# Unread constant products on TensorE at the start and in the slots of two stages, shorter rotary tables, a rotated bank ring

## The reference

```python
# q, k, v: (4, 8, 576, 64); each head of each batch:
q_rot, k_rot = rotate(q), rotate(k)                  # rotary embedding with cos and sin
scores = scale * q_rot @ k_rot.T
attn = exp(scores - max(scores)); attn = attn / (sum(attn) + 1e-9)
attn_out = attn @ v
# x: (4, 576, 512), the heads side by side
h = x.transpose(0, 2, 1) @ U @ V                     # U: (576, 32), V: (32, 576)
u = x + h.transpose(0, 2, 1)
out = u + relu(u @ w_ch1) @ w_ch2                    # 512 -> 2048 -> 512
```

## Time and profile before

| | us |
|---|---|
| median of 3 runs | 759.92 (759.8 to 761.0) |
| profiled execution, device time | 758.6 |
| its span, first to last instruction | 756.8 |
| PE busy | 714.9 |
| POOL, ACT, DVE busy | 464.9, 439.3, 405.3 |

### The profile page before, as it was taken

The page is one execution under the profiler, slowest core; times in us unless marked ns, Lnnn a source line. Parts: engine busy times, 40 slices in busy tenths (PEclk is TensorE's granted clock), DMA queues, the critical chain, the costliest instruction groups (busy, mean ns, idle before and its releaser), DMA issues.

```text
span 756.8 us, 12306 instructions
## 1 busy us (share of the span) xinstructions
PE 714.9 (94%) x4292; PEld 644.6 (85%) x4292; DVE 405.3 (54%) x675; ACT 439.3 (58%) x948; POOL 464.9 (61%) x338
## 2 busy tenths in 40 slices
PE   3999977899999989999999999989999999999998
PEld 3888875798998879899999988879899889999986
DVE  4799977655556775443454466666565441112111
ACT  2788865666666665565565665657656443334341
POOL 3998846485849663674855957638432446565653
PEclk9999999999999999999999999999999999999999
DMA  7976682627383528448275274372612254434341
GB/s 206 239 215 183 174 250 74 199 87 227 102 254 105 167 94 240 155 130 258 81 213 183 96 197 146 117 211 69 169 70 98 70 195 137 166 127 169 128 169 72
DMA packets 73964, 118.11 MB, mean 156 GB/s; under 512 B 27056, under 2 KB 27184, under 8 KB 72112
## 3 DMA queue, kind: packets, MB, share of 16 engines
q1 hardware_dynamic: 73472, 116.68, 50.9%
q10 hardware_dynamic: 432, 0.66, 0.3%
HBM read 80.45 MB, written 9.44 MB: 119 GB/s over the span
## 4 chain that ended last, share of the span: by engine, by line
PE 75%; DVE 9%; ACT 7%; issue 5%; DMA 1%; POOL 1%; SPq 0%; POOLq 0%; ACTq 0%; DVEq 0%
PE ps L1129 25%; PE ps L1145 23%; PE ps L1043 8%; PE ps L1029 8%; PE ps L1063 6%; DVE negmax L863 3%; ACT prob L711 2%; PE ps L1056 1%; DVE ptl L872 1%; PE ps L1021 1%; DMA raw<-in_qk 1%; DVE pth L876 1%; ACT low L728 1%; PE ps L1086 1%; ACT pth L722 1%
## 5 line engine op out<-in xcount | busy, mean ns | idle before, releaser
L647 POOL TENSOR_TENSOR w2l<-w2u,w2h 128x512 fp32r<-128x512 f32 x96 | 123.8, 1290 | 227.4 <-ACT w2h L775 227.4
L964 DVE SCALAR_TENSOR_TENSOR htl<-ps,hth 128x384 fp32r<-128x384 f32 x96 | 53.5, 558 | 184.8 <-ACT hth L782 184.5
L863 DVE TENSOR_REDUCE negmax<-ps 128x1 f32<-128x576 f32 (+1 forms) x160 | 120.2, 751 | 56.4 <-PE ps L1029 46.6
L722 ACT ACTIVATE pth<-ps 128x512 fp32r<-128x512 f32 x156 | 87.8, 567 | 87.1 <-PE ps L1063 85.3
L711 ACT ACTIVATE prob<-ps,negmax 128x576 f32<-128x576 f32 (+1 forms) x160 | 118.1, 738 | 33.9 <-DVE negmax L863 32.4
L1129 PE MATMUL ps<-ub,w1h 128*128 128x384 f32 x384 | 132.3, 344 | 1.8 <-DVE utl L955 1.8
L1129 PE MATMUL ps<-ub,w1l 128*128 128x384 f32 x384 | 129.4, 337 | 0.0
L1129 PE MATMUL ps<-utl,w1h 128*128 128x384 f32 x384 | 129.2, 336 | 0.0
L641 POOL TENSOR_TENSOR w1l<-w1u,w1h 128x512 fp32r<-128x512 f32 x96 | 123.6, 1288 | 6.7 <-ACT w1h L771 6.7
L782 ACT ACTIVATE hth<-ps 128x384 fp32r<-128x384 f32 x96 | 47.1, 491 | 137.6 <-PE ps L1129 137.3
L1029 PE MATMUL ps<-stack 128*128 128x288 f32 x620 | 114.4, 307 | 9.3 <-ACT prob L711 9.0
(11 more groups left out here) (80 smaller groups left out, 1128.1 us busy)
## 6 DMA issues: line engine op xcount, KB each, us to landing
w1u<-in_w SPq DMA_DIRECT2D x96, 256.0 KB, 2.6
w2u<-in_w SPq DMA_DIRECT2D x96, 256.0 KB, 2.7
stack<-raw SPq DMA_DIRECT2D x60, 288.0 KB, 4.5
raw<-in_qk SPq DMA_DIRECT2D x14, 1152.0 KB, 5.4
stack<-raw SPq DMA_DIRECT2D x60, 144.0 KB, 3.9
v2u<-in_v SPq DMA_DIRECT2D x16, 320.0 KB, 3.8
ubu<-scratch_u SPq DMA_DIRECT2D x18, 256.0 KB, 3.7
out<-ubu SPq DMA_DIRECT2D x18, 256.0 KB, 2.2
```

Source lines behind the costliest of these rows:

```text
L647: nc.gpsimd.tensor_tensor(w2l[:, at], w2u[:, at], w2h[:, at], ALU.subtract).then_inc(w2_lo, 1)
L722: nc.scalar.activation(pt_of(g)[0][rows, keys, queries], source, ACT.Copy).then_inc(pt_hi, 1)
L863: nc.vector.tensor_reduce(negmax[0:WT[t], t:t + 1], scores_of(n, WT[t]), AX.XY, ALU.max, negate=True).then_inc(maxed, 1)
```

## The change

It has five parts. (1) Ahead of everything TensorE waits for a DVE memset of `hsum` and makes six 128x512 products of it into bank 7, which nobody reads; the wait for the identity comes after them. (2) In slots 1 to 7 and 47 to 55 two products of the identity with itself (128x128, plain fp32) are made into the first score bank, after the wait for that bank and ahead of the scores, which overwrite them. (3) The tables come as one DMA of 64 partitions, and DVE copies them to the other 64. SP issues q and k of round 1 and v of round 0 at once, with no wait, ahead of head 1's operands; k of round 1 has a semaphore of its own. POOL begins the product of round 1's q as soon as the tables are doubled and q is loaded, and waits for DVE's two splits after that product. (4) `RING_MIXED` is rotated by one bank. (5) LAGGED is 51.

```diff
+WARM_UP = 6
+FILLED, FILLERS = (*range(1, 8), *range(47, 56)), 2
-MERGED, LAGGED, MLP_FROM = 46, 50, 56
+MERGED, LAGGED, MLP_FROM = 46, 51, 56
-RING_ALONE, RING_MIXED, RING_MERGED = (4, 5, 6, 7), (4, 5, 6, 7, 2, 3), (6, 7)
+RING_ALONE, RING_MIXED, RING_MERGED = (4, 5, 6, 7), (5, 6, 7, 2, 3, 4), (6, 7)
             sp.dma_start(raw[:, 0, :, 0], qk[0][:, :, 0]).then_inc(raw_loaded[0], 16)
-            sp.wait_ge(raw_loaded[0], 16)
             sp.dma_start(raw[:, 1, :, 0], qk[1][:, :, 0]).then_inc(raw_loaded[1], 16)
+            sp.dma_start(raw[:, 1, :, 1], qk[1][:, :, 1]).then_inc(next_k, 16)
+            load_v(0)
             sp.wait_ge(lo_split[1], 1)
             stack_k(sp, 0, 1)
             sp.wait_ge(lo_split[0], 1)
             stack_q(sp, 0, 1)
-            sp.dma_start(raw[:, 1, :, 1], qk[1][:, :, 1]).then_inc(first_loaded, 16)
-            load_v(0)
             load_v(1)
                 link(nc.gpsimd.tensor_tensor(both, both, tables[:, :, :], ALU.mult))
+                if r == 1 and which == 0:
+                    for i in range(2):
+                        pool.wait_ge(lo_split[i], 1)
                 nc.gpsimd.tensor_tensor(both[:, 0], both[:, 0], both[:, 1], ALU.add).then_inc(roped[which], 1)
-            pool.wait_ge(tables_loaded, 32)
-            for which in range(2):
-                pool.wait_ge(lo_split[which], 1)
+            pool.wait_ge(tables_twice, 1)
-            act.dma_start(tables[:, 0], cos).then_inc(tables_loaded, 16)
-            act.dma_start(tables[:, 1], sin).then_inc(tables_loaded, 16)
+            act.dma_start(tables[0:D], trig).then_inc(tables_loaded, 16)
-            dve.wait_ge(tables_loaded, 32)
+            nc.vector.memset(hsum[:, :], 1.0).then_inc(filled, 1)
+            dve.wait_ge(tables_loaded, 16)
+            nc.vector.tensor_copy(tables[D:P], tables[0:D]).then_inc(tables_twice, 1)
+            dve.wait_ge(tables_twice, 1)
+            pe.wait_ge(filled, 1)
+            for _ in range(WARM_UP):
+                nc.tensor.matmul(ps[:, 7 * BANK:8 * BANK], hsum[:, 0:P], hsum[:, :], start=True, stop=True)
             pe.wait_ge(ident_loaded, 16)
+            def fill(at):
+                for _ in range(FILLERS):
+                    nc.tensor.matmul(ps[:, at:at + P], ident[:, :], ident[:, :], start=True, stop=True)
                 at = 2 * BANK * (n % 2 if n < MERGED else 0)
+                if n in FILLED:
+                    fill(at)
```

More of the change, by code:

```diff
@@ L284, in _down_read, with build @@
         eng.wait_ge(e["down_done"], i + 1 - p)
-def build(nc, qk, v, cos, sin, identity, u4, v4, w, scratch_u, out):
+def build(nc, qk, v, trig, identity, u4, v4, w, scratch_u, out):
     out = out.rearrange("b s d -> (b s) d")
@@ L335, in build @@
         vmraw = lu[:, :, :].rearrange("p x n -> p (x n)")[:, 0:S]
-        tables_loaded, ident_loaded = sem("tables_loaded"), sem("ident_loaded")
+        tables_loaded, ident_loaded, filled = sem("tables_loaded"), sem("ident_loaded"), sem("filled")
+        next_k, tables_twice = sem("next_k"), sem("tables_twice")
         first_loaded, mix_loaded, mix_consts = sem("first_loaded"), sem("mix_loaded"), sem("mix_consts")
@@ L366, in _engines @@
 def _engines(nc, e):
-    (qk, v, cos, sin, identity, u4, v4, w, scratch_u, out, bank_of, before, left) = (e[x] for x in (
-        "qk v cos sin identity u4 v4 w scratch_u out bank_of before left").split())
+    (qk, v, trig, identity, u4, v4, w, scratch_u, out, bank_of, before, left) = (e[x] for x in (
+        "qk v trig identity u4 v4 w scratch_u out bank_of before left").split())
     (ps, ident, tables, raw, first, stack, v2u, v2, prob, pth, ptl, low, xt, negmax, sums, inv, xn, xh, xl, hsum, hs, us, vs,
@@ L372, in _engines @@
          "uth utl w1h w1u w1l w2h w2u w2l hth htl res uraw vmraw pt_buffers").split())
-    (tables_loaded, ident_loaded, first_loaded, mix_loaded, mix_consts, zeroed, raw_loaded, v_loaded, first_rope,
+    (tables_loaded, ident_loaded, filled, next_k, tables_twice, first_loaded, mix_loaded, mix_consts, zeroed, raw_loaded, v_loaded, first_rope,
      chain, roped, qk_hi, lo_split, v_hi, v_split, stacked, scored, maxed, expd, transposed, pt_hi, pt_lo, pv_done,
@@ L377, in _engines @@
      relu_lo, down_done, acc_done, added, res_loaded, stored) = (e[x] for x in (
-         "tables_loaded ident_loaded first_loaded mix_loaded mix_consts zeroed raw_loaded v_loaded first_rope "
+         "tables_loaded ident_loaded filled next_k tables_twice first_loaded mix_loaded mix_consts zeroed raw_loaded v_loaded first_rope "
          "chain roped qk_hi lo_split v_hi v_split stacked scored maxed expd transposed pt_hi pt_lo pv_done "
@@ L605, in prepare @@
                     if r == 1:
-                        pool.wait_ge(first_loaded, 32)
+                        pool.wait_ge(next_k, 16)
                     rope(r, 1)
@@ L1212 @@
     s = np.sin(freqs).T.astype(np.float32)
-    c = np.concatenate([c] * 4, axis=0)
-    s = np.concatenate([-s, s] * 2, axis=0)
+    c = np.concatenate([c] * 2, axis=0)
+    s = np.concatenate([-s, s], axis=0)
     root = np.float32(D ** -0.25)
-    cos = np.ascontiguousarray(c * root)
-    sin = np.ascontiguousarray(s * root)
-    arrays = {"qk": qk, "v": vp, "cos": cos, "sin": sin, "identity": np.eye(P, dtype=np.float32),
+    trig = np.ascontiguousarray(np.stack([c * root, s * root], axis=1))
+    arrays = {"qk": qk, "v": vp, "trig": trig, "identity": np.eye(P, dtype=np.float32),
               "u4": u4, "v4": v4, "w": w}
@@ L1223 @@
     out = nc.dram_tensor("out", (B, S, DM), my.dt.float32, kind="ExternalOutput").ap()
-    build(nc, aps["qk"], aps["v"], aps["cos"], aps["sin"], aps["identity"], aps["u4"], aps["v4"], aps["w"],
+    build(nc, aps["qk"], aps["v"], aps["trig"], aps["identity"], aps["u4"], aps["v4"], aps["w"],
           scratch_u, out)
```

## The result

The changed kernel takes 763.09 us (median of 9 runs, 762.2 to 764.9), the kernel before 760.04 us beside it (median of 9, 759.4 to 762.1). The ratio is 1.005, with a 95% interval of 1.0036 to 1.0063: 3 us slower, where 753.5 us was forecast. The profiled execution took 762.95 us, its span is 761.1 us. That of the kernel before (758.6 us) was 1.4 us under its median, so the profiles lie 4.3 us apart where the medians lie 3.05 us apart.

A forecast was written before the change was run, and what follows sets the result against it. TensorE bounds from 142 us, DVE from about 37 us to slot 46, TensorE's low clock before. 758.6 - 2.7 (start) - 3.1 (middle) = 752.8 us; as a median 754.1, taken as 753.5, range 749.5 to 757.5.

The forecast's parts named there:

- The clock in slots 1 to 7: Head 0's slots: TensorE runs at 2.4 instead of 1.2 GHz, so a slot takes 1.68 instead of 2.78 us.
- The slower rival, C: Slots 1 to 7 stay at 1.2 GHz, seven pairs cost 6.2 us: 761 us, 763 with POOL in the way; chance 0.07.
- the loads: At the start: one table DMA less brings products 1 and 0 forward by 0.8 us.
- the middle: Slots 46 to 55: 2.9 + 0.5 - 0.3 = 3.1 us gained, between 1 and 4.
- POOL against DVE: Start: POOL's early product delays a DVE step, first maximum at 14.2 instead of 11.7 us, 2.5 us given back.
- The price of the unread products: On TensorE: a pair costs 0.44 us at 2.4 GHz, twice that at 1.2; the six at the start some 9 us.
- The gain at the high clock: Start to slot 12: 5.2 us gained in all, 1.4 of it by the first maximum, before POOL's delay.
- POOL isn't late: Heads 2 and 3: after DVE's splits POOL does what it did before, less the 2.62 us product of q.
- Slot 46, the ring: TensorE's 3.20 us idle wait for bank 4 goes; the maximum of slot 47 moves from 103.17 to 100.3, 2.9 us.
- Slots 47 to 55: DVE is nearer to being the bound, TensorE's room takes most pairs; 0.3 us charged for all nine.
- LAGGED: Slot 51: the 0.69 us `hsum` step moves from ahead of the maximum to behind it, 0.5 us gained.
- start: Up to slot 12: 2.7 us gained with POOL's product in DVE's way, 5.2 without.

The follow-up runs named there:

- e1: The changed kernel with POOL's waits for DVE's two splits put back ahead of POOL's first product; 760.69 us, ratio 1.0001 to the kernel before.
- e5: e1 with nine instead of six unread products at the start; 754.54 us, ratio 0.9935.
- e10: e7 without the pairs of unread products in slots 1 to 7, so nine products at the start and no pairs; 754.8 us, ratio 0.9919.
- e11: e6 with the pairs of unread products in slots 47 to 55 alone; 757.85 us, ratio 0.9969.
- e4: The changed kernel without the six products at the start and the pairs in slots 1 to 7; late pairs stay; 758.77 us, ratio 0.9985.
- e7: e5 without the pairs of unread products in slots 47 to 55; 754.26 us, ratio 0.9930.
- e6: The changed kernel without any unread products and with POOL's waits as in e1; 754.0 us, ratio 0.9935.
- e2: The kernel before with RING_MIXED rotated by one bank and nothing else; 756.03 us, ratio 0.9949.
- e8: e2 with LAGGED = 51; 755.59 us, ratio 0.9952.
- e9: The changed kernel, POOL's early product included, with eleven instead of six products at the start; 758.32 us, ratio 0.9969.
- e12: e7 with the load of round 2 issued behind head 2's operands instead of ahead of them; 761.68 us, ratio 1.0013.

## Why the prediction was wrong

**The clock in slots 1 to 7** is the step that failed. The sum took it that a clock once raised would stay up, though the same text had TensorE idle from about 9 us to the first scores and quoted 3.20 idle us ahead of a fall. In the profile it rose at 6.96 us and fell at 13.79. e1 shows that the fall needs no help from POOL, e5 that closing the gap with three more products prevents it, and e10 that these nine without the pairs don't: the clock then falls at 15.68 us. The step thus lacked a condition: the unread products must reach up to the first scores, and head 0's slots must be filled (one of e1's twelve executions kept the clock without the first). Only slots 1 to 5 ran at the low clock, with a pair in each, 15.80 us from maximum 0 to 5 instead of 11.05. The slower rival, C, described exactly this, at 763 us with POOL in the way; 763.09 was measured. That it meets the number so closely is partly luck: it charged 6.2 us for seven cold pairs, where five cost 4.8, and took off 0.8 us for the loads and 3.1 for the middle, where 0.2 or so and 2.3 came. It had been given 0.07. What is wrong is that chance: nothing in the rows of the kernel before showed the high clock surviving such idleness, and the timing that I worked out myself put it there.

**POOL against DVE** was right in kind, place and nearly in size: L843 or L848 stretched beside L582, first maximum at 14.82 us (14.2 forecast), 2.3 to 2.4 us by e11 against e4 (2.5 forecast).

**The price of the unread products** was nearly right: 0.85 us a pair at 1.2 GHz in the chain above (1.15 in slots 1 and 2), 0.45 at 2.4 GHz (105.55 us in the chain of the changed kernel), against 0.88 and 0.44. The six took 8.14 us, against some 9. The Trainium skill's four passes ("FP8 and Floating Point Precision", "TensorE Precision Notes") fit. Each product is recorded as two instructions, and one product of 512 columns, two of them, takes 1.70 us at 1.2 GHz. Four passes at the price of a 288-column product at 1.2 GHz (0.97 / 4 us) would be 4 x 512/288 x 0.24 = 1.7 us.

**The gain at the high clock** was too large as well. With the clock held (e7) maximum 0 to 8 gains 2.8 us where 5.2 - 1.4 = 3.8 was summed (a slot of head 0 takes 1.8 us and not 1.68), and slot 10 then waits for head 2's operands. "POOL isn't late" was argued from POOL's own steps and is right for them. It left out what follows POOL's last split: the order of SP's queue, and the time from issue to landing, 5.4 to 9.1 us here. That took a further 1.8 us off in e7.

**The loads**: 0.2 us or so instead of 0.8. The first maximum is at 12.81 and 13.05 us in e6 and e11, and with the old loads at 13.12, 12.97 and 13.18 us (before, e2, e8). DVE's first product began at 5.92 instead of 6.02 us, waiting for k and no longer for the table, and products 0 then follow on DVE without a wait for q. The term counted bytes and not the last arrival.

**Slot 46, the ring**: 2.9 us forecast; 2.8 in the changed kernel (3.50 against 6.30 us from maximum 46 to 47), 2.9 in e2. Right.

**Slots 47 to 55**: the charge of 0.3 us was wrong, 2.3 us were measured (e11). DVE was taken as the bound with TensorE's slack to spare, but from slot 46 to 51 the chain goes through TensorE's parts (the chain of the changed kernel has L1059, L1108 and the pair itself in a row), and a later DVE step slid into POOL's. **LAGGED**: not told apart from nothing.

Of the sum, then: start -2.7 forecast, +6.2 measured (at slot 0 +1.7: POOL +2.4, less what the loads and the six products bring; slots 1 to 12 +4.5); middle -3.1 forecast, -2.3 measured; the 615 us after it as long as before.

## What to carry to other kernels

Work that only keeps a clock up is worth what it prevents only if it reaches, without a gap, to the work it is for: follow the clock to the first useful product before counting on it, and price the filler at the low clock too, where it sits on the chain. When a stage gets faster, look for the next arrival in the stage (here the DMA of head 2's operands) up to its landing and not to its issue. And look first at where a ring of buffers starts its count: turning one tuple gave 2.9 us at no cost, and with the loads, LAGGED and POOL's old order it is the whole of e6, at 754.0 us. No version with unread products is faster than that clear of the noise.

## What the runs showed of the hardware

A DVE step with two SBUF operands and a step of POOL exclude each other: the two splits took 3.84 instead of 1.59 us, a step of 0.76 us took 3.06, and POOL's own step grew from 2.62 to 3.11 us. The same `hs` step took 0.77 us where it fell between two steps of POOL (e6), 1.92 us where it began just behind the start of one (e11, changed), and 2.83 us at most. This is the lock of the Trainium skill's "SBUF — State Buffer", section "SBUF: two separate sides", and the rows agree with it.

The same program keeps or loses its high clock from one execution to the next: e1 spread from 753.1 to 762.7 us with mean granted clocks of 1.000 to 0.987, e10 from 751.7 to 757.0. The kernel before took 756.8 to 757.8 us wherever the mean was 0.998 and 760.0 to 762.4 us where it was 0.989. One profile alone would have called e10 faster than e6 by 1.8 us, where its median is 0.8 us higher. Five of the fourteen profiles (e1, e7, e8, e11, e12) have one more fall of 3.41 us between 597 and 607 us; from maximum 57 to the end of the span these take 615.3 to 616.5 us, the others 613.6 to 614.6.

DMAs of 288 KB into `stack` took 4.3 to 9.1 us to land, longest close behind a load of 1152 KB on the same queue: 9.1 us with the load issued 2.2 us before (changed), 8.7 with 3.9 (e9), 6.9 and 5.4 with 4.6 and 4.5 (e7, e5), 4.3 with 9.5 (e12).
